# One-core attention with two dense blocks: how the second input is split, where the root mean square is reduced, and the order of several queues

## The reference, cut to what matters

```python
def _attn_ref(q, k, v, cap):                  # (2, 12, 448, 64)
    scores = cap * np.tanh(q @ k.T / sqrt(64) / cap)
    attn = softmax(scores)
    return attn @ v                           # then laid out as x: 896 tokens x 768

def _moe_ref(x, w_in, w_out):                 # 768 -> 2048 -> 768
    h = x @ w_in
    return np.maximum(0.01 * h, h) @ w_out

def _moe2_ref(x, w_gate, w_val, w_out, rms_g):   # 768 -> 1536 -> 768
    rms = np.sqrt(np.mean(x * x, axis=-1, keepdims=True) + 1e-06)
    xn = x / rms * rms_g
    g = xn @ w_gate
    silu = g * (1.0 / (1.0 + np.exp(-g)))
    return (silu * (xn @ w_val)) @ w_out
```

## Time and profile before

| | us |
|---|---|
| median of the runs (lowest to highest) | 589.04 (588.64 to 589.37) |
| the profiled execution, its own time | 589.37 |
| its span, first to last instruction | 587.2 |
| TensorE matmuls busy | 568.0 (97%) |
| VectorE busy | 384.8 (66%) |
| GpSimd busy | 274.0 (47%) |
| ScalarE busy | 259.5 (44%) |

### The profile page before, as it was taken

The page is one execution under the profiler, slowest core; times in us unless marked ns, Lnnn a source line. Parts: engine busy times, 40 slices in busy tenths (PEclk is TensorE's granted clock), DMA queues, the critical chain, the costliest instruction groups (busy, mean ns, idle before and its releaser), DMA issues.

```text
span 587.2 us, 7730 instructions
## 1 busy us (share of the span) xinstructions
PE 568.0 (97%) x2805; PEld 494.4 (84%) x2805; DVE 384.8 (66%) x515; ACT 259.5 (44%) x426; POOL 274.0 (47%) x236
## 2 busy tenths in 40 slices
PE   4999999999999999999999979999999999999997
PEld 2555565578999999999999969999999999999997
DVE  4259898589888776335975595988888878611120
ACT  4877787214333353335643545434444444311110
POOL 1006555387855652334653574765687865100000
PEclk9999999999999999999999999999999999999999
DMA  6145442121211131110210011412211114100001
GB/s 165 53 140 164 129 132 63 33 72 55 107 55 54 55 123 66 55 54 28 81 54 28 1 55 54 162 55 77 86 54 55 55 54 135 55 27 28 28 27 55
DMA packets 29861, 41.48 MB, mean 71 GB/s; under 512 B 17024, under 2 KB 18816, under 8 KB 29824
## 3 DMA queue, kind: packets, MB, share of 16 engines
q1 hardware_dynamic: 29824, 40.99, 21.5%
HBM read 38.15 MB, written 2.80 MB: 70 GB/s over the span
## 4 chain that ended last, share of the span: by engine, by line
PE 86%; DMA 5%; DVE 4%; issue 2%; POOL 1%; ACT 1%; SPq 0%; DVEq 0%; POOLq 0%; ACTq 0%
PE ps L1288 40%; PE ps L1330 19%; PE ps L1407 15%; PE ps L1239 6%; PE ps L1220 2%; PE ps L1243 1%; DMA sums<-x_raw 1%; DMA recips<-recip 1%; PE ps L1224 1%; DMA w_raw<-in_w_in 1%; DMA capc<-in_cap 1%; DVE x_raw L815 1%; POOL w_lo L480 1%; ACT probs L576 1%; DMA recip_row<-recips 1%
## 5 line engine op out<-in xcount | busy, mean ns | idle before, releaser
L480 POOL TENSOR_TENSOR w_lo<-w_raw,w_hi 128x384 fp32r<-128x384 f32 x92 | 108.2, 1180 | 131.7 <-ACT w_hi L593 131.4
L1288 PE MATMUL ps<-x_hi,w_hi 128*128 128x448 f32 x420 | 155.1, 369 | 5.4 <-issue 4.4
L1288 PE MATMUL ps<-x_hi,w_lo 128*128 128x448 f32 x420 | 154.1, 367 | 0.0
L1288 PE MATMUL ps<-x_lo,w_hi 128*128 128x448 f32 x420 | 154.1, 367 | 0.0
L480 POOL TENSOR_TENSOR w_lo<-s_sum,w_hi 128x384 fp32r<-128x384 f32 x80 | 90.2, 1134 | 43.0 <-ACT w_hi L593 42.8
L1288 PEld LDWEIGHTS ps<-x_hi,w_hi 128*128 128x128 f32 x420 | 79.4, 189 | 14.7 <-issue 6.4
L1288 PEld LDWEIGHTS ps<-x_hi,w_lo 128*128 128x128 f32 x420 | 79.4, 189 | 6.4
L1288 PEld LDWEIGHTS ps<-x_lo,w_hi 128*128 128x128 f32 x420 | 79.4, 189 | 6.2
L593 ACT ACTIVATE w_hi<-s_sum 128x384 fp32r<-128x384 f32 x80 | 41.6, 523 | 82.5 <-PE ps L1288 74.4
L1239 PE MATMUL ps<-probs,v_ones 128*128 128x448 f32 x144 | 56.3, 541 | 1.1 <-DVE x_raw L815 1.1
L593 ACT ACTIVATE w_hi<-w_raw 128x384 fp32r<-128x384 f32 x92 | 47.3, 515 | 14.6 <-PE ps L1288 14.1
(11 more groups left out here) (136 smaller groups left out, 926.7 us busy)
## 6 DMA issues: line engine op xcount, KB each, us to landing
w_raw<-in_w_out SPq DMA_DIRECT2D x24, 384.0 KB, 3.0
w_raw<-in_w_in SPq DMA_DIRECT2D x16, 384.0 KB, 3.7
qk_raw<-in_qk SPq DMA_DIRECT2D x12, 480.0 KB, 4.4
w_raw<-in_w_gate SPq DMA_DIRECT2D x12, 384.0 KB, 2.9
w_raw<-in_w_val SPq DMA_DIRECT2D x12, 384.0 KB, 3.7
v_ones<-in_v SPq DMA_DIRECT2D x12, 224.0 KB, 3.3
recip_row<-recips SPq DMA_DIRECT2D x12, 224.0 KB, 3.3
v_raw<-in_w_out SPq DMA_DIRECT2D x4, 384.0 KB, 5.9
```

The costliest lines, as they stand in the source:

```text
L480: pool.tensor_tensor(w_lo[:, c], source, w_hi[:, c].bitcast(F32), ALU.subtract).then_inc(w_lo_done, 1)
L1288: last = pe.matmul(ps[:, base(s) + BANK_OF[j], 0:S], w[:, w_c], x[:, xs(j, c)], start=(j in (P1, P5, P7, P6) and c == 0 and w is w_hi and ...
```

## The change

It has these parts:

- **Second half of the rows.** VectorE first scales B22 and B21 from PSUM into SBUF buffers (`second_half`); T2 and T4 are then differences of two SBUF buffers, the upper parts are made by ScalarE from SBUF, and the six lower parts of B22 and B21 move from VectorE to GpSimd.
- **Mean square.** The last row of squares is no longer added by GpSimd; TensorE adds it with seven more matmuls. The 14 matmuls stand before P4 of unit 8, and the spreading of the inverse root before P5 of unit 9.
- **Gated stage.** Units 8 and 9 go through the same loop as the others. VectorE now waits for `r_bc` inside unit 8, and `s_parts(10)` and `take_p5(9)` come behind the gates of unit 8.
- **Order of sums.** In every unit all four `s_part` stand before `take_p5`; before, two stood before it and two after. In unit 3 the clearing of `sq_acc` then stands between them and `take_p5`.
- **Attention.** The load of `cap` goes before that of the first q and k. TensorE's first scores of each pair wait for both parts of q and k. SyncE's order in the loop over pairs changes, and the last `reciprocal` goes before the last but one `normalise`.

```diff
-            load_qk(0)
             sp.dma_start(capc[:, 0:1], cap.partition_broadcast(128)).then_inc(cap_in, 16)
+            load_qk(0)
...
             for p in range(PAIRS):
-                spread_sums(p)
+                if p > 0:
+                    store_recip(p - 1)
+                if p + 3 < PAIRS:
+                    load_qk(p + 3)
+                if p > 0:
+                    load_recip_row(p - 1)
                 if p + 2 < PAIRS:
                     load_v(p + 2)
-                if p + 4 < PAIRS:
-                    load_qk(p + 4)
                 if p < 4:
                     load_raw(p, w_in[p])
-                store_recip(p)
-                load_recip_row(p)
+                spread_sums(p)
...
+            weight_lo(widx(U1, P6))
+            y_lo(B22, 1)
+            y_lo(B21, 1)
+            weight_lo(widx(U1, P3))
+            weight_lo(widx(U1, P2))
+            y_lo(B22, 2)
+            y_lo(B21, 2)
+            weight_lo(widx(U1, P4))
             add_squares(KH + 1)
-            add_squares(KH + 2)
...
+            reciprocal(PAIRS - 1)
             normalise(PAIRS - 2)
-            reciprocal(PAIRS - 1)
...
-                    s_part(s + 1, P5)
-                    s_part(s + 1, P7)
+                    s_parts(s + 1)
...
+            def second_half(m):
+                wait_row(dve, m)
+                scaled(B22, m, 1)
+                scaled(B21, m, 0)
...
-                from_bank(y_source(T2, c), c, 1, y_source(T1, c)).then_inc(y_done, 1)
+                dve.tensor_tensor(y_source(T2, c), y_source(B22, c), y_source(T1, c), ALU.subtract).then_inc(y_done, 1)
...
+            second_half(KH + 2)
+            t2_t3(2)
+            t4(2)
+            take_p5(U1)
+            for blk in (T2, T3, T4):
+                y_lower(blk, 2)
             s_parts(U1 + 1)
...
+            for s in range(U1, UNITS):
+                if U1 < s < UNITS - 1:
+                    s_parts(s + 1)
                 if s > U1:
-                    gate_sum(s)
+                    take_p5(s)
                 take_p7(s)
+                if s == U1:
+                    mean_square()
...
+                if s == U1:
+                    inverse_root()
+                    dve.wait_ge(r_bc_done, 2)
...
+            pe.wait_ge(acc_done, 2 * (KD - 1))
+            pe.wait_ge(sq_done, 2 * KD)
+            for t in range(TT):
+                pe.matmul(ps[:, 1, t:t + 1], sq_acc[:, t * 128:(t + 1) * 128], ones[:, 0:1], start=True, stop=False)
+                last = pe.matmul(ps[:, 1, t:t + 1], g[:, 22 * S + t * 128:22 * S + (t + 1) * 128], ones[:, 0:1],
+                                 start=False, stop=True)
+            last.then_inc(ss_done, 1)
             product(s, P4)
             product(s + 1, P1)
+            pe.wait_ge(rinv_done, 1)
...
+            product(s + 1, P5)
+            pe.wait_ge(r_bc_done, 2)
+            for j in (P7, P6, P3, P2, P4):
                 product(s + 1, j)
```

More of the change, by code:

```diff
@@ L300, in build @@
         y_t1 = [r_bc[:, cols(1)], u2[1][:, :], g_tile(27)]
-        y_t4 = [extra[:, :], g_tile(24), g_tile(25)]
+        y_b22 = [a_t[1][:, :], g_tile(24), g_tile(28)]
+        y_b21 = [extra[:, :], g_tile(25), g_tile(29)]
+        y_t4 = [extra[:, :], g_tile(20), g_tile(21)]
         def y_source(blk, c):
-            return {B11: y_b11, T3: y_b11, T1: y_t1, T2: y_t1, T4: y_t4}[blk][c]
+            return {B11: y_b11, T3: y_b11, T1: y_t1, T2: y_t1, B22: y_b22, B21: y_b21, T4: y_t4}[blk][c]
         def square_tile(m, b):
@@ L553, in value_lo_half @@
                     lower.then_inc(v2_lo_half, 1)
-            for s in range(U1 + 2, UNITS):
+            for s in range(U1 + 1, UNITS):
                 for j in range(7):
@@ L709, in _ @@
             squares(2)
+            y_hi(B22, 1)
             y_hi(B21, 1)
             weight_hi(widx(U1, P6))
-            y_hi(B22, 1)
             y_hi(T2, 1)
@@ L762, in split_act @@
                 act.activation(tiles(split_hi[tt % 2][:, f0 * 128:f1 * 128], 128), src, ACT.Copy).then_inc(split_hi_done, 1)
-            silu(U1, 1)
-            silu(U1, 0)
-            weight_hi(widx(U1 + 2, P3))
-            silu(U1 + 1, 1)
-            weight_hi(widx(U1 + 2, P2))
-            silu(U1 + 1, 0)
-            weight_hi(widx(U1 + 2, P4))
-            for s in range(U1 + 2, UNITS - 1):
-                keep_p1(s)
-                for j in range(5):
+            for s in range(U1, UNITS - 1):
+                if s > U1 + 1:
+                    keep_p1(s)
+                for j in range(0 if s > U1 else 5, 5):
                     weight_hi(widx(s + 1, j))
@@ L1061, in _ @@
                     y_lower(T1, 1)
+                if i == N1 + 2:
+                    second_half(KH)
                 if i == N1 + 3:
                     t2_t3(0)
-                if i == N1 + 5:
-                    plain_lower(B22, 0)
-                    plain_lower(B21, 0)
+                if i == N1 + 6:
                     t4(0)
-                if i == N1 + 6:
                     y_lower(T2, 0)
@@ L1082, in _ @@
             y_lower(T1, 2)
-            for c in (1, 2):
-                t2_t3(c)
-                plain_lower(B22, c)
-                plain_lower(B21, c)
-                t4(c)
-                if c == 2:
-                    take_p5(U1)
-                for blk in (T2, T3, T4):
-                    y_lower(blk, c)
+            second_half(KH + 1)
+            t2_t3(1)
+            t4(1)
+            for blk in (T2, T3, T4):
+                y_lower(blk, 1)
+            second_half(KH + 2)
+            t2_t3(2)
+            t4(2)
+            take_p5(U1)
+            for blk in (T2, T3, T4):
+                y_lower(blk, 2)
             s_parts(U1 + 1)
@@ L1273, in x_ready @@
                 elif s in (U1, U1 + 1):
-                    if j == B11:
+                    if j in (B11, B22, B21):
                         pe.wait_ge(y_lo_pool, y_pool_count[j, c])
```

138 lines of the change are left out of this document (32 added, 106 removed).

## The result

The changed kernel takes 604.2 us (median; 602.2 to 607.5), the kernel before 588.96 on the same chip: ratio 1.0264, 95% interval [1.0218, 1.031]. The forecast was 596.9 us with a range of 592 to 601.5. The sign is right and the size is not: 15.2 us were lost where 7.9 were expected, and the time lies outside the range.

What follows compares the result with a forecast made beforehand. It took TensorE's work plus its idle places as the bound; 5.3 - 3.4 + 6.5 + 0.4 + 0.2 - 0.9 + 0.4 - 0.6 = +7.9 on 589.37 gave 597.3 us profiled, 596.9 by median, range 592 to 601.5.

Steps and rivals of the forecast that it cites:

- (8): Attention: sums issued behind v and, for four pairs, a weight panel in SyncE's new order; +0.4 us (0 to 2).
- (2): Before P4 of unit 8: old stall and its low clock go, longer sum over partitions is added; -3.4 us (-3.4 to -2.7).
- own sign of being wrong: Forecast wrong if the wait before P3 of unit 8 or 9 is below 2 us, or attention loses over 2 us.
- (1): End of second projection: P3 of unit 8 waits 3.8 us for take_p5(8), plus 1.5 low clock; +5.3 us (0 to 6.2).
- (3): Before P5 of unit 9: mean square and root hidden behind P4 and P1, spreading 0.7 us as before; 0.
- (4): P3 of unit 9: new wait of 5.0 us for take_p5(9), plus 1.5 low clock; +6.5 us (1.6 to 8.0).
- (5): Other units, four sums before take_p5: covered, except +0.4 us (0 to 1.4) in units 2 and 3 together.
- (6): Middle of the second projection: extra scalings and lower parts make step 20's lower parts late; +0.2 us (0 to 1).
- (7): Start: with cap loaded first, the first scores are ready 0.9 us earlier (1.4 earlier to 0.4 later).
- the small transfers bind: Rival, chance 0.08: each pair's sums land 2 us later or more, stalling attention in three groups of pairs; 601.4 us.
- (9): End of attention: earlier last reciprocal shortens the 1.06 us stall, the one before moves later; net -0.6 us (-1 to +0.5).
- steady units stay as they are: Sign in the later profile: steady units stay at 63 matmuls each without a wait.

Runs made afterwards that it cites:

- second profile: The changed kernel profiled again without any edit: profiled execution 605.74 us, median 604.7 us, ratio 1.0246.
- after_t_from_psum: The changed kernel with T2 and T4 of c = 1 and 2 read from PSUM with the gain, as before: 603.6 us, ratio 1.0213.
- after_sums_10_late: The changed kernel with the four sums of unit 10 moved behind take_p5 of unit 9: 599.6 us, ratio 1.0142.
- sums_ahead_hidden: The kernel before with only the sums of units 3 to 7 put ahead of take_p5 of the unit before: 590.95 us, ratio 0.9994.
- first profile: The first profile of the unedited changed kernel: its execution took 609.18 us, 5 us above the median.
- sync_order_alone: The kernel before with only SyncE's new order in attention: 597.3 us, ratio 1.0083.
- sync_sums_before_v: The kernel before with SyncE's new order in attention, but a pair's sums issued ahead of v and the weight panel: 589.3 us, ratio 0.9979.
- after_old_sync_order: The changed kernel with SyncE's old order in attention: 600.2 us, ratio 1.0132.
- start_and_reciprocal: The kernel before with cap loaded ahead of the first q and k and the last reciprocal ahead of the normalisation before it: 588.1 us, ratio 0.9946.
- before_take_p7_first: start_and_reciprocal with take_p7 of unit 8 also moved ahead of the four sums of unit 9: 585.5 us, ratio 0.9894 against the kernel before.
- after_take_p5_first: The changed kernel with take_p5 of unit 8 ahead of the last column tile's T2, T3, T4, and keep_p1 ahead of T2's high part: 609.1 us, ratio 1.0282.

## Why the prediction was right in sign and short in size

The step that failed is (8), SyncE's order: it was priced at +0.4 us, at most 2, and cost 5.0 and 6.4. With attention as forecast the second profile would stand at 599.7 us, inside the range. The rest is mainly a missing term in (2) and a slower pace of the units that the prediction did not have. The prediction's own sign of being wrong, more than 2 us lost in attention, came true. By its steps, in the profile of after unless said otherwise.

(1) *Wait for take_p5(8)*: 2.4 us against 3.8, inside its bounds (0 to 4.7) but below the 3 to 5 given as its sign; the low clock came, 6.42 us for 24 matmuls (4.9 at full clock), 1.5. The mechanism, T2 to T4 slowed by GpSimd, was shown by after_t_from_psum. They took 1.2 to 1.5 us, not 1.5 to 1.66, and T4 for c = 1 took 0.62, where the hand count had it behind a GpSimd instruction. GpSimd had no gap from 340.9 to 352 us, as assumed; the argument "in the last group before there was no gap" does not fit the trace of before, where it idled 2.2 us before 339.19 and 1.5 us before 341.70.

(2) *Old stall gone*: the wait is gone, and the sum took 3.04 us, 1.6 more. **A term was missing**: the clock fell a second time, directly behind the one-column matmuls (6.01 us for 18 matmuls and the seven of the spreading, 4.4 at full clock: 1.6 us). The step came out at -1.7 instead of -3.4. I had counted them by their own time alone. The earlier trace rows could not warn: there 14 of them ran just behind a stretch of low clock and no second one followed. That the shorter wait in (1) hid about as much as this term cost is luck.

(3) *Spreading*: nothing, as predicted.

(4) *Wait for take_p5(9)*: 5.5 us against 5.0, and 1.8 us of low clock against 1.5 (54 matmuls in 12.94 us, 11.1 at full clock). Right, with four contended sums as argued, and shown by after_sums_10_late. Its lower bound was added wrongly: 3.5 + 4 x 0.5 + 0.6 is r + 6.1, a stall of 1.8 us and not 1.6, which changes nothing in the forecast.

(5) *Sums ahead of take_p5*: 1 us in units 2 and 3 (0.4 predicted) by sums_ahead_hidden and the second profile. In the first profile the wait was 1.9 us and the clock fell; the program is the same, so that differs between executions. In steady units it costs nothing while nothing else is late; just behind a catching-up stretch it costs 1.6 us (unit 10 in after_sums_10_late).

(6) *Middle*: 0 for +0.2. (7) *Start*: -1.1 for -0.9.

(8) *SyncE's order*: **the step that failed**. +5.0 and +6.4 us in attention where I wrote +0.4, with 2 as the upper bound. I took 1.1 us of head start for `v` and the panel from the end of the products, and overlooked that `load_recip_row` stands ahead of them with its wait. The row that priced it was there: 4.4 us for a small transfer behind 1.1 MB. The rival "the small transfers bind" had this mechanism at 601.4 us and got 0.08; it was right, and with the 0.4 it put attention at +4.9. The measured loss is made of waits of 1.9 and 2.1 us (2.0 and 3.6 in the second profile) where there was one of 1.1, and one stretch of low clock in each. sync_order_alone, sync_sums_before_v and after_old_sync_order show the cause from both sides.

(9) *End of attention*: the stall of 1.06 us is gone as predicted; the waits of units 0 and 1 fall from 1.9 us (0.2, 1.1, 0.7) to 1.3 (0.4, 0.6, 0.3), 0.6 less.

**Not foreseen: the pace of the units.** I wrote that steady units stay as they are. Two kernels whose units 2 to 7 are the same program, start_and_reciprocal and then before_take_p7_first, ScalarE's copy of P1 once per unit:

```profile
166.17 0.55 ACT L599 ACTIVATE p<-ps 128x448 f32<-128x448 f32 x1 [1.29 <-PE ps L1288]
178.94 0.55 ACT L599 ACTIVATE p<-ps 128x448 f32<-128x448 f32 x1 [1.30 <-PE ps L1288]
```

```profile
166.43 0.55 ACT L599 ACTIVATE p<-ps 128x448 f32<-128x448 f32 x1 [1.33 <-PE ps L1288]
179.45 0.55 ACT L599 ACTIVATE p<-ps 128x448 f32<-128x448 f32 x1 [1.33 <-PE ps L1288]
```

12.77 and 13.02 us for the same 63 matmuls, at a granted clock of 1.00 in both and with no wait of TensorE between. What sets the pace no run shows. In the first profile of after both the later hidden units and the ten gated ones had the slower pace, 1 and 2.5 us; in the second the hidden ones only. That, and the longer wait in unit 2 with its low clock, is what sets the first profile above the second.

Sum of the misses for the second profile, which is near the median: start and attention +5.7, units 0 to 7 +2.1, to P3 of unit 8 -1.5, from there to P3 of unit 9 +2.2, the end and outside the span 0: 8.5 us beyond the 7.9. Of the 2.1, some 1.1 us are the slower pace and 0.6 the sums ahead of `take_p5` beyond their forecast.

## What to carry to other kernels

A small transfer that a chain of work waits for goes ahead of large ones on its queue, and where an order is changed the waits of the instructions moved past count as much as their bytes. Work inserted before the instruction that frees TensorE is priced at its contended length (1.2 to 1.6 us here, not 0.6), and the cheapest cure was to move the one short instruction that TensorE waits for ahead of the four long ones (some 3 us for two exchanged lines, less than the stall of 3.4 with its low clock), where nothing else was late. Price a wait with the low clock that may follow, and look for other light stretches of TensorE beside idle ones.

## What the runs showed of the hardware

- TensorE runs the same back-to-back matmuls (448 columns) at one of two paces at full granted clock: 12.77/63 = 0.2027 us and 13.02/63 = 0.2067 us each. In the 16 profiles the pace changed only behind a matmul that started some 0.06 us late or more, or behind a stretch of low clock, and then held for the rest of the section, up to 133 us. It was the slow one in the hidden units of 7 of the 16 profiles and in the gated units of 3, whichever order the kernel had. What decides it stays open.
- The low clock does not follow a wait by its length alone. A wait of 3.4 us was followed by it in before and not in sums_ahead_hidden; the same wait of 2.4 us before P3 of unit 8 was followed by it in after and not in after_sums_10_late or after_old_sync_order. In attention one of 1.7 us was (after_take_p5_first) and one of 2.8 us was not (after_sums_10_late).
- This differs between executions of one kernel, and it makes the larger part of their spread of up to 6 us. Of the 24 executions of before beside sync_order_alone, the three with a mean granted clock of 1.00 took 587.9 to 590.3 us and the seven with 0.991 took 592.2 to 594.2. A stretch of 3.4 us at half the clock is 0.003 of that mean and 1.7 us.
- It also follows stretches in which TensorE issues only one-column matmuls without idling: behind 28 recorded ones in all six profiles where these ran at the full clock (at 361.9 us in after). Behind 14 it came in one profile of six, at 351.6 us in before_take_p7_first, with a wait of 0.4 us ahead of them; in four of the other five they ran 1.3 to 2.1 us behind a stretch of low clock.
- A transfer of 3.5 KB landed in 2.1 us with nothing ahead, and in 4.5 to 5.0 behind 832 KB issued within the 2 us before it; 224 KB issued 2 us ahead cost nothing.
